# A spectral mixer with a feed-forward network: eight places for the first units' rows, the last pairs' table in six transfers, two splits moved

## The chip, the cores and the metric

The kernel runs on one core of a Trainium2 chip. The metric is the device time of one execution in microseconds. PE is the matmul engine (TensorE), DVE VectorE, ACT ScalarE, POOL GpSimd and SP SyncE, which only issues transfers. ACT and POOL issue transfers as well.

## The reference

Two parts follow each other. The first takes x (4 batches, 3008 positions, 256 channels) through a real Fourier transform over the positions, mixes the channels with a complex matrix, shrinks the result and goes back. The second is a feed-forward network with 2048 hidden units on the 12032 rows.

```python
X = np.fft.rfft(x, axis=1)
Yr = Xr @ w_r - Xi @ w_i + b_r
Yi = Xr @ w_i + Xi @ w_r + b_i
Y = sign(Y) * maximum(abs(Y) - 0.01, 0)      # real and imaginary part each
y = np.fft.irfft(Y, n=3008, axis=1)          # as 12032 rows of 256
h = y @ w_in
out = (maximum(h, 0) + alpha * minimum(h, 0)) @ w_out
```

## The kernel before

A position is 32 a + b with a below 94 and b below 32, and the transform is done in two steps. Every float32 operand of a matmul is split into two parts, a "hi" (a copy rounded to fp32r) and a "lo" (what is left), and three matmuls (hi hi, hi lo, lo hi) stand for one product. The hi is a copy on ACT or DVE, the lo a subtraction on DVE or POOL (`rest`).

The work of one batch:

- **forward1(s)**, 16 units of two values of b: the first transform step, three matmuls of 512 columns. DVE splits x (`split_x`: a cast to x_hi, then x_lo). ACT copies the result out of PSUM (`copy_fwd`, L816) and stores it to a scratch tensor in HBM (`store_fwd`, L363). The place in SBUF that it is copied to is given by `out_place` and `out_rows`; a place is written again only when the store that last read it has landed.
- **forward2(p)**, 24 pairs: the second step on 128 rows loaded back from the scratch (`load_pair`, pair_raw), which needs all of the batch's stores. ACT makes pair_hi (`split_pair`), DVE pair_lo (`rest_pair`). The stationary operand's counterpart is the table tw_parts, one for three pairs: ACT makes its hi (`split_tw`, L825), POOL its lo (`rest_tw`, L1332).
- **mixing(p)**: 12 matmuls with the channel matrix mixw, from spec_hi (ACT, `split_spec`) and spec_lo (DVE, `rest_spec`). POOL negates a part of spec_lo.
- add_bias (DVE), find_above (ACT), shrink (DVE), then shr_hi (ACT, `split_shrunk`) and shr_lo (DVE, `rest_shrunk`); **inverse2(p)** with the table itw, copied to inv_sb by ACT (`copy_inv`) and stored.
- **inverse1(u)**: the last step, which makes y_hi and y_lo in SBUF, the input of the feed-forward network.

The network runs over 24 tiles of some 502 rows, 16 steps each (hidden, then output two steps later). Batches 1 to 3 of the first part are put between its steps. Only batch 0 has a stretch of its own, before the tiles: 16 units of forward1 up to 23 us, the 24 pairs from 32 to 96 us, then some rest of inverse work, and the tiles from 109 us on.

The order of the instructions on every engine is written out by hand, engine by engine (sync from L369, tensor, scalar, vector, gpsimd), and semaphores tie them. No planner is at work. In batch 0's stretch the order on each engine is a loop over k from -1 to 22, and in iteration k:

- PE: forward2(k+1), mixing(k), inverse2(k-2);
- ACT: copy_inv(k-3), split_spec(k+1), find_above(k-1), split_pair(k+3), split_shrunk(k-1), then at k = 0, 3, ... 18 split_tw(k/3+1) and at k = 2, 5, ... 20 split_itw;
- DVE: add_bias(k-1), rest_spec(k+1), shrink(k-1), rest_pair(k+3), rest_shrunk(k-1), then at odd k from 3 to 17 a piece of a weight's split, and at k = 19 and 21 split_x of units 16 and 17, which belong to batch 1;
- POOL: negate(k+1), then rest_tw or rest_itw.

The hand-over from forward1 to the pairs: PE runs 29 filler matmuls (`stay_warm_early`, L732, 0.24 us each, whose result nobody reads) after unit 15. SP waits for the stores of all places and then loads pairs 0 to 3. Places for the rows of units 0 to 15 are taken in turn from six (OUT_FIRST): two in staging, two in g_raw, biased and shrunk.

The table of the last two pairs: pairs 22 and 23 are not taken through HBM at the end of the first part, but multiplied directly with their rows of the inverse matrix, spread over a zeroed tile (`last_raw`, in rows). POOL zeroes it when unit 7's x is split and fills it with small transfers (`load_last`, L1391): for each of two pairs e and six values b, 4 rows of 94 numbers, 12 transfers in all. DVE then makes g_hi and g_lo from it (L1242), and after that mixw_lo and the first two pair_lo, in this order.

Of the kernel before, what the change touches and what calls it, by code (L numbers as in the profile page):

```python
# [15 lines left out]
NA, NB = 94, 32  # L16
PAIRS = (NA // 2 + 1) // 2
ROWS = 4 * PAIRS
GROUPS = PAIRS // 3
# [29 lines left out]
S_HEAD = NB // 2  # L49
# [4 lines left out]

OUT_RING, OUT_HEAD = 2, 4

OUT_FIRST = 6
HEAD_V = 3

PAIRS_END = 2  # L60

HEAD_ROWS = 4 * (PAIRS - PAIRS_END)
# [67 lines left out]
def mixer_kernel(nc, x, w_r, w_i, b_r, b_i, w_in, w_out, alpha, dft, idft, twiddles, out):  # L130
    with ExitStack() as ctx:
# [35 lines left out]
        biased = sb("biased", [P, 2, DIM])  # L167
        above = sb("above", [P, 2, DIM])
        low = sb("low", [P, 1])
        shrunk = sb("shrunk", [P, 2, DIM])  # L170
        shr_hi, shr_lo = (sb(f"shr_{h}", [P, 2, DIM], F32R) for h in ("hi", "lo"))
        inv_sb = sb("inv_sb", [P, 3, DIM])


        rows = sb("rows", [P, HEAD_V, 2 * DIM])
# [26 lines left out]
        def ffw_raw(w):  # L202
            return turned[:, w % 2, :, :, :, :].rearrange("p k b h e -> p (k b h e)")[:, 0:4 * DIM]

        h_ps = ctx.enter_context(nc.psum_tensor("h_ps", [P, 2, 512], F32))
# [29 lines left out]
        last_zero, last_hi_done, last_lo_done, end_hi_done, end_lo_done, last_loaded = (  # L235
            sem(n) for n in ("last_zero", "last_hi_done", "last_lo_done", "end_hi_done", "end_lo_done", "last_loaded"))
# [87 lines left out]
        def out_rows(s):  # L324
            k = out_place(s)
            if k >= OUT_HEAD:
                return (biased, shrunk)[k - OUT_HEAD][0:ROWS, :, :].rearrange("p q d -> p (q d)")
            return staging[:, k, :] if k < OUT_RING else g_raw[0:ROWS, k - OUT_RING, :]

        def stores_before(s, k):  # L330
# [36 lines left out]
        def _(sp):  # L367
# [29 lines left out]
            def load_pair(p):  # L397
                g, j = divmod(p, PAIRS)
                if p >= 4:
                    sp.wait_ge(pair_lo_done, p - 3)  # L400
                if j < 4:
                    for k in range(OUT_FIRST):
                        sp.wait_ge(fwd_stored[k], stores_before(S_HEAD * (g + 1), k))
                sp.dma_start(pair_raw[:, p % 4, :], fwd_pairs[g, :, j, :]).then_inc(pair_loaded[p % 4], 16)
# [90 lines left out]
            for f in range(TILES):  # L495
                for m in range(STEPS):
# [21 lines left out]
                    p = p_unit(f, m, 0)  # L518
# [3 lines left out]
                    p = p_unit(f, m, 2)  # L522
                    if p is not None and p % 3 == 0:
                        load_table(p // 3 + 1)
                    p = p_couple(f, m, 6)
# [17 lines left out]
        def _(pe):  # L543
# [186 lines left out]
            def stay_warm_early(count, ps):  # L730
                for n in range(count):
                    pe.matmul(ps, dft_hi[:, :], x_hi[:, 1, :], start=True, stop=True)  # L732
# [11 lines left out]
            pe.wait_ge(hi_const, 1)  # L744
            for s in range(S_HEAD):
                forward1(s)
            stay_warm_early(29, h_ps[:, 1, :])
            for k in range(-1, PAIRS - 1):
                forward2(k + 1)
                if k == 0:  # L750
# [32 lines left out]
            for f in range(TILES):  # L783
                for m in range(STEPS):
# [8 lines left out]
                    p = p_unit(f, m, 0)  # L793
                    if p is not None:
                        forward2(p)
                    p = p_couple(f, m, 5)
# [3 lines left out]
                    p = p_couple(f, m, 2)  # L800
                    if p is not None:
                        mix_couple(p)
                    q = f * STEPS + m - LAG
# [6 lines left out]
        def _(act):  # L810
# [7 lines left out]
            def split_tw(t):  # L818
                if t < GROUPS:
                    act.wait_ge(table_loaded[t % 2], 16 * (t // 2 + 1))  # L820
                else:
                    act.wait_ge(table_loaded[0], 16 * (GROUPS // 2 + t - GROUPS + 1))
                if t >= 2:
                    act.wait_ge(spec_mm, 3 * (t - 1))
                act.activation(tw_parts[:, t % 2, :, 0, :], table_place(t)[:, 0, :].rearrange("p (k c) -> p k c", k=3),  # L825
                               ACT.Copy).then_inc(tw_hi_done, 1)
# [64 lines left out]
            def find_above(p):  # L891
                act.wait_ge(biased_done, p + 1)
                if p >= 1:
                    act.wait_ge(shrunk_done, p)
                act.activation(above[:, 0, :], biased[:, p % 2, :], ACT.Relu, bias=low[:, :]).then_inc(above_done, 1)  # L895
# [80 lines left out]
            for k in range(-1, PAIRS - 1):  # L976
                if k >= 3:
                    copy_inv(k - 3)
                split_spec(k + 1)
                if k >= 1:  # L980
                    find_above(k - 1)
                if 2 <= k + 3 < PAIRS:
                    split_pair(k + 3)
                if k >= 1:
                    split_shrunk(k - 1)
                if k >= 0 and k % 3 == 0 and k // 3 + 1 < GROUPS:
                    split_tw(k // 3 + 1)
                if k >= 0 and k % 3 == 2 and k // 3 + 1 < GROUPS:
                    split_itw(k // 3 + 1)
            for p in (PAIRS - 2, PAIRS - 1):  # L990
# [18 lines left out]
            for f in range(TILES):  # L1009
                for m in range(STEPS):  # L1010
                    q = f * STEPS + m
# [3 lines left out]
                    p = p_unit(f, m, 0)  # L1015
# [9 lines left out]
                    p = p_couple(f, m, 5)  # L1025
                    if p is not None:
                        copy_couple(p)
                    p = p_couple(f, m, 3)
# [5 lines left out]
                    p = p_unit(f, m, -3)  # L1034
                    if p is not None:
                        split_pair(p)
                    p = p_unit(f, m, 0)
# [8 lines left out]
                    p = p_unit(f, m, 0)  # L1046
# [16 lines left out]
        def _(dve):  # L1063
# [3 lines left out]
            def split_x(s, both):  # L1067
                x_arrived(dve, s)
                if s >= 2:
                    dve.wait_ge(fwd_mm, s - 1)  # L1070
                elif s == 0:
                    dve.wait_ge(x_zero, 2)
                dve.tensor_copy(x_hi[0:NA, s % 2, :], x_place(s)).then_inc(x_hi_done, 1)  # L1073
                if both:
                    dve.wait_ge(x_hi_done, s + 1)
                    rest(x_lo[0:NA, s % 2, :], x_place(s), x_hi[0:NA, s % 2, :]).then_inc(x_lo_done, 1)
# [156 lines left out]
            for s in range(S_HEAD):  # L1233
# [4 lines left out]
                if s == 6:  # L1238
                    dve.wait_ge(hi_const, 2)
                    rest(idft_parts[0:ROWS, 1, :], idft_raw[0:ROWS, 0:NA], idft_parts[0:ROWS, 0, :]).then_inc(const_split, 1)  # L1240
            dve.wait_ge(last_loaded, 16 * PAIRS_END * 2 * HEAD_V)
            dve.tensor_copy(flat(g_hi), last_raw).then_inc(last_hi_done, 1)  # L1242
            dve.wait_ge(last_hi_done, 1)
            rest(flat(g_lo), last_raw, flat(g_hi)).then_inc(last_lo_done, 1)
# [5 lines left out]
            for k in range(-1, PAIRS - 1):  # L1250
                if k == 1:
                    dve.wait_ge(bias_loaded, 32)
                if k >= 1:
                    add_bias(k - 1)
                rest_spec(k + 1)
                if k >= 1:
                    shrink(k - 1)
                if 2 <= k + 3 < PAIRS:
                    rest_pair(k + 3)
                if 1 <= k < PAIRS - 2:  # L1260
                    rest_shrunk(k - 1)
                if 3 <= k < 19 and k % 2 == 1:
                    split_ffw((k - 3) // 8, (k - 3) % 8 // 2)
                if k in (19, 21):
                    split_x(S_HEAD + (k - 19) // 2, True)
            for p in (PAIRS - 2, PAIRS - 1):
                add_bias(p)
                rest_shrunk(p - 1)
# [61 lines left out]
        def _(pool):  # L1330
# [54 lines left out]
                rest(wout_lo[:, w, :, :].rearrange("p m e -> p (m e)"), ffw_raw(w)[:, 2 * DIM:4 * DIM],  # L1385
                     wout_hi[:, w, :, :].rearrange("p m e -> p (m e)")).then_inc(wout_lo_done, 1)

            def load_last(e, b):

                row = HEAD_V * 2 * DIM  # L1390
                pool.dma_start(bass.AP(rows[:, :, :].tensor, b * row + (e * 2 * HEAD_V + b) * NA, [[32 * row, 4], [1, NA]]),  # L1391
                               idft[HEAD_ROWS + 4 * e:HEAD_ROWS + 4 * e + 4, 0:NA]).then_inc(last_loaded, 16)

            pool.memset(idft_parts[ROWS:P, 1, :].bitcast(F32), 0.0).then_inc(lo_zero, 1)
            pool.wait_ge(lo_zero, 1)
# [3 lines left out]
            pool.wait_ge(x_lo_done, 8)  # L1399
            pool.memset(last_raw, 0.0).then_inc(last_zero, 1)  # L1400
            pool.wait_ge(last_zero, 1)
            for e in range(PAIRS_END):
                for b in range(2 * HEAD_V):
                    load_last(e, b)
            rest_tw(0)
            rest_itw(0)
            for k in range(-1, PAIRS - 1):
# [102 lines left out]
```

## Time and profile before

| | us |
|---|---|
| median of 3 runs | 1375.19 |
| lowest, highest | 1373.89, 1375.62 |
| the profiled execution | 1378.68 |
| its span | 1376.9 |
| PE busy in the span | 1360.3 (99%) |
| DVE busy | 1026.8 (75%) |
| ACT busy | 763.7 (55%) |
| POOL busy | 327.9 (24%) |

The span runs from the first instruction of the profiled execution to its last; 1.8 us of its time lie around it. Busy shares are means over the whole: the first 110 us, batch 0's stretch, look different from the tiles.

### The profile page before, as it was taken

The page shows a single profiled execution, that of the slowest core. Times are in us where ns is not written, and L with a number is a line of the kernel's source. Part 1 is how long each engine was busy: PE and PEld are TensorE (multiplying, and loading weights), DVE is VectorE, ACT ScalarE, POOL GpSimd, SP SyncE. Part 2 cuts the span into 40 slices and gives each one's busy share as a digit, 9 for nine tenths or more (in the row PEclk, how much of TensorE's full clock was granted, in tenths as well). Part 3 has the DMA queues.
Part 4 walks back from the last instruction along what each step waited for, and adds up shares of the span by engine and source line. Part 5 has one row for each costly group of instructions (what it writes and reads, how often), then busy time and mean ns, then how long its engine had stood idle before and what let it go on. Part 6 is the DMA issues. An engine that isn't in the chain of part 4 may idle for free.

```text
span 1376.9 us, 21744 instructions
## 1 busy us (share of the span) xinstructions
PE 1360.3 (99%) x6933; PEld 1158.1 (84%) x6933; DVE 1026.8 (75%) x1892; ACT 763.7 (55%) x1711; POOL 327.9 (24%) x370
## 2 busy tenths in 40 slices
PE   8999999999999999999999999999999999999997
PEld 5998888888888888888888888888888888888886
DVE  7787788898866768989866668888886566566654
ACT  4776566666544555756644446666564444444443
POOL 4534542232201422323300332233220000000000
PEclk9999999999999999999999999999999999999999
DMA  8554523231211541323312333223211021102101
GB/s 264 168 173 139 173 68 92 70 92 54 52 44 46 144 117 58 86 70 83 78 30 50 87 108 84 72 74 81 85 43 44 26 50 39 25 26 50 27 15 16
DMA packets 174896, 106.82 MB, mean 78 GB/s; under 512 B 112442, under 2 KB 150586, under 8 KB 174783
## 3 DMA queue, kind: packets, MB, share of 16 engines
q1 hardware_dynamic: 170344, 101.58, 27.4%
q10 hardware_dynamic: 3959, 3.70, 0.8%
q8 instruction: 56, 0.92, 0.3%
q14 instruction: 57, 0.47, 0.1%
q0 software_dynamic: 480, 0.16, 0.1%
HBM read 67.89 MB, written 37.49 MB: 77 GB/s over the span
## 4 chain that ended last, share of the span: by engine, by line
PE 93%; DVE 2%; ACT 2%; issue 1%; POOL 1%; DMA 1%; SPq 0%; POOLq 0%; ACTq 0%; DVEq 0%
PE out_ps L546 39%; PE h_ps L546 38%; PE work_ps L546 10%; PE work_ps L657 2%; PE work_ps L589 2%; PE work_ps L659 1%; ACT above L895 1%; PE work_ps L590 1%; DVE shrunk L1135 1%; POOL rows L1391 0%; SPq L381 0%; ACT shr_hi L901 0%; DMA rows<-in_idft_dram 0%; DMA rows<-in_x_dram 0%; DVE biased L1127 0%
## 5 line engine op out<-in xcount | busy, mean ns | idle before, releaser
L934 ACT ACTIVATE rows<-h_ps 128x502 f32<-128x502 f32 (+1 forms) x384 | 225.3, 587 | 510.3 <-PE h_ps L546 510.3
L1166 DVE SCALAR_TENSOR_TENSOR g_raw<-rows,keep,h_ps 128x502 f32<-128x502 f32 (+1 forms) x384 | 280.3, 732 | 264.6 <-ACT rows L934 261.3
L546 PE MATMUL out_ps<-g_hi,wout_hi 128*128 128x502 f32 (+1 forms) x768 | 305.0, 397 | 0.2
L546 PE MATMUL h_ps<-y_hi,win_hi 128*128 128x502 f32 (+1 forms) x768 | 300.0, 391 | 1.2 <-DVE g_raw L1166 1.0
L546 PE MATMUL out_ps<-g_hi,wout_lo 128*128 128x502 f32 (+1 forms) x768 | 299.8, 390 | 0.0
L546 PE MATMUL h_ps<-y_lo,win_hi 128*128 128x502 f32 (+1 forms) x768 | 299.7, 390 | 0.0
L546 PE MATMUL out_ps<-g_lo,wout_hi 128*128 128x502 f32 (+1 forms) x768 | 299.0, 389 | 0.0
L546 PE MATMUL h_ps<-y_hi,win_lo 128*128 128x502 f32 (+1 forms) x768 | 298.9, 389 | 0.0
L1065 DVE TENSOR_TENSOR g_lo<-g_raw,g_hi 128x502 fp32r<-128x502 f32 (+1 forms) x384 | 268.4, 699 | 1.8 <-ACT g_hi L943 1.4
L943 ACT ACTIVATE g_hi<-g_raw 128x502 fp32r<-128x502 f32 (+1 forms) x384 | 237.0, 617 | 6.7 <-DVE g_raw L1166 6.2
L546 PEld LDWEIGHTS h_ps<-y_hi,win_hi 128*128 128x128 f32 x768 | 145.0, 189 | 32.1 <-issue 2.0
L546 PEld LDWEIGHTS h_ps<-y_hi,win_lo 128*128 128x128 f32 x768 | 144.4, 188 | 30.7
L546 PEld LDWEIGHTS out_ps<-g_hi,wout_lo 128*128 128x128 f32 x768 | 144.8, 189 | 29.9
L546 PEld LDWEIGHTS h_ps<-y_lo,win_hi 128*128 128x128 f32 x768 | 144.7, 188 | 29.5
L546 PEld LDWEIGHTS out_ps<-g_hi,wout_hi 128*128 128x128 f32 x768 | 145.0, 189 | 23.1 <-DVE g_lo L1065 1.0
L546 PEld LDWEIGHTS out_ps<-g_lo,wout_hi 128*128 128x128 f32 x768 | 145.5, 189 | 22.2
L1332 POOL TENSOR_TENSOR back_lo<-inv_sb,back_lo 128x256 fp32r<-128x256 f32 x61 | 54.4, 892 | 414.0 <-ACT back_lo L920 413.9
L1354 POOL TENSOR_TENSOR room<-room 128x128 f32<-128x128 f32 x72 | 60.0, 834 | 322.6 <-DVE room L1089 322.6
L1332 POOL TENSOR_TENSOR x_lo<-x_raw,x_hi 94x512 fp32r<-94x512 f32 x44 | 59.0, 1340 | 83.0 <-DVE x_hi L1073 83.0
L546 PE MATMUL work_ps<-mixw_hi,spec_hi 128*128 128x256 f32 x216 | 61.5, 285 | 0.0
L546 PE MATMUL work_ps<-mixw_lo,spec_hi 128*128 128x256 f32 x216 | 61.0, 282 | 0.0
L546 PE MATMUL work_ps<-mixw_hi,spec_lo 128*128 128x256 f32 x216 | 60.9, 282 | 0.0
(177 smaller groups left out, 2032.2 us busy)
## 6 DMA issues: line engine op xcount, KB each, us to landing
pair_raw<-fwd_scratch SPq DMA_DIRECT2D x96, 128.0 KB, 2.2
rows<-inv_scratch SPq DMA_DIRECT2D x61, 192.0 KB, 2.4
table<-in_twiddles_dram SPq DMA_DIRECT2D x28, 384.0 KB, 3.5
inv_scratch<-inv_sb SPq DMA_DIRECT2D x36, 256.0 KB, 2.2
x_raw<-in_x_dram SPq DMA_DIRECT2D x56, 160.0 KB
fwd_scratch<-staging SPq DMA_DIRECT2D x46, 192.0 KB, 2.1
inv_sb<-inv_scratch SPq DMA_DIRECT2D x122, 64.0 KB, 2.3
out_dram<-turned SPq DMA_DIRECT2D x124, 40.0 KB, 1.8
```

What stands on the lines that cost most here:

```text
L546: mm = pe.matmul(ps, lhs, rhs, start=(first and n == 0), stop=(last and n == len(terms) - 1), **kw)
L589: pe.matmul(both, hi, tw.rearrange("p w c -> p (w c)"), start=True, stop=False, skip_group_check=True)
L590: mm = pe.matmul(both[:, 0:P], lo, tw[:, 0, :], start=False, stop=True, skip_group_check=True)
L657: pe.matmul(i_bank(u)[:, b * 2 * NA:(b + 1) * 2 * NA], back_hi[:, v % 2, d], parts, start=b == 0, stop=False, skip_group_check=True)
L659: pe.matmul(i_views(u)[0], back_lo[:, v % 2, h * P:(h + 1) * P], idft_rest[:, :, :], start=False, stop=True, skip_group_check=True).then_i ...
L895: act.activation(above[:, 0, :], biased[:, p % 2, :], ACT.Relu, bias=low[:, :]).then_inc(above_done, 1)
L934: act.activation(negpart[:, q % 2, 0:size], h_ps[:, q % 2, 0:size], ACT.Relu, scale=-1.0).then_inc(negpart_done, 1)
L943: act.activation(g_hi[:, q % 3, 0:size], g_raw[:, q % 2, 0:size], ACT.Copy).then_inc(g_hi_done, 1)
L1065: return dve.tensor_tensor(dst, whole, hi.bitcast(F32), ALU.subtract)
L1166: dve.scalar_tensor_tensor(g_raw[:, q % 2, 0:size], negpart[:, q % 2, 0:size], keep[:, m:m + 1], h_ps[:, q % 2, 0:size], ALU.mult, ALU.add ...
L1332: return pool.tensor_tensor(dst, whole, hi.bitcast(F32), ALU.subtract)
L1354: pool.tensor_tensor(spec_sum, spec[:, :, 0, :], spec[:, :, 1, :], ALU.add).then_inc(sum_done, 1)
```

## The change

Five edits, all in batch 0's stretch.

```diff
-OUT_FIRST = 6
+OUT_FIRST = 8
@@ out_rows
-                return (biased, shrunk)[k - OUT_HEAD][0:ROWS, :, :]...
+                return (biased, shrunk, above, inv_sb)[k - OUT_HEAD][0:ROWS, 0:2, :]...
@@ load_pair
-                if j < 4:
+                if j == 0:
                     for k in range(OUT_FIRST):
                         sp.wait_ge(fwd_stored[k], stores_before(S_HEAD * (g + 1), k))
@@ tensor
-            stay_warm_early(29, h_ps[:, 1, :])
+            stay_warm_early(27, h_ps[:, 1, :])
@@ scalar, the loop over k
+                if k >= 0 and k % 3 == 0 and k // 3 + 1 < GROUPS:
+                    split_tw(k // 3 + 1)
                 if 2 <= k + 3 < PAIRS:
                     split_pair(k + 3)
                 if k >= 1:
                     split_shrunk(k - 1)
-                if k >= 0 and k % 3 == 0 and k // 3 + 1 < GROUPS:
-                    split_tw(k // 3 + 1)
@@ vector
-            dve.wait_ge(last_loaded, 16 * PAIRS_END * 2 * HEAD_V)
+            dve.wait_ge(last_loaded, 16 * 2 * HEAD_V)
...
-                if k in (19, 21):
-                    split_x(S_HEAD + (k - 19) // 2, True)
+                if k in (18, 20):
+                    split_x(S_HEAD + (k - 18) // 2, True)
@@ gpsimd
-            def load_last(e, b):
+            def load_last(b):
                 row = HEAD_V * 2 * DIM
-                pool.dma_start(bass.AP(rows[:, :, :].tensor, b * row + (e * 2 * HEAD_V + b) * NA, [[32 * row, 4], [1, NA]]),
-                               idft[HEAD_ROWS + 4 * e:HEAD_ROWS + 4 * e + 4, 0:NA]).then_inc(last_loaded, 16)
+                pool.dma_start(bass.AP(rows[:, :, :].tensor, b * row + b * NA, [[32 * row, 4], [2 * HEAD_V * NA, PAIRS_END], [1, NA]]),
+                               idft[HEAD_ROWS:HEAD_ROWS + 4 * PAIRS_END, 0:NA].rearrange("(e r) a -> r e a", e=PAIRS_END)
+                               ).then_inc(last_loaded, 16)
@@
-            for e in range(PAIRS_END):
-                for b in range(2 * HEAD_V):
-                    load_last(e, b)
+            for b in range(2 * HEAD_V):
+                load_last(b)
```

Units 0 to 15 take their places in turn from eight; the two new ones lie in above and in the first two thirds of inv_sb. SP checks the places' stores once per batch, ahead of pair 0, as it issues in order. Units 16 and up keep the four and two places that they had. The last pairs' table moves the same 48 rows in six transfers of eight rows. PE has two fillers fewer. On ACT the table's split of an iteration stands ahead of the pair's and of shr_hi. The x splits of units 16 and 17 are done one iteration earlier.

## Rows read from the trace of the kernel before

**Rows 1.** Busy time by windows: length, engines' busy time (instructions), granted clock, DMA share, GB/s.

```profile
29.90:31.90 2.00, 0.00 (x0) 0.03 (x1) 2.00 (x3) 0.76 (x2) 0.44 (x1) 1.00 0.91 219
31.90:36.00 4.10, 4.10 (x17) 3.81 (x18) 1.70 (x5) 2.12 (x7) 0.93 (x2) 0.52 0.90 308
...
90.00:96.00 6.00, 5.09 (x41) 4.78 (x40) 4.72 (x13) 3.69 (x12) 2.30 (x4) 1.00 0.40 128
...
150.00:700.00 550.00, 550.00 (x2854) 472.87 (x2853) 447.42 (x818) 324.58 (x737) 158.32 (x179) 1.00 0.30 79
```

**Rows 2.** PE's waits over the whole run: total us, times, longest.

```profile
PE h_ps L546 <- DVE pair_lo L1065: 2.1, 1, 2.1
...
PE h_ps L546 <- POOL tw_parts L1332: 0.8, 2, 0.5
```

**Rows 3.** The chain that ended last, 0 to 70 us: start, us, what.

```profile
15.14 6.59 POOL rows L1391 x11
21.73 4.91 DMA rows<-in_idft_dram
...
27.44 2.04 DVE g_lo L1065
...
66.10 0.62 PE h_ps L546 x6
66.72 1.47 PE out_ps L546 x12
```

**Rows 4.** Timeline, 22 to 40 us: start, us, engine, line, what [idle before].

```profile
22.69 0.39 PE L546 MATMUL work_ps<-x_hi,dft_lo 128*128 128x512 f32 x1
...
22.93 6.90 PE L732 MATMUL h_ps<-x_hi,dft_hi 128*128 128x512 f32 x29
24.29 0.59 ACT L816 ACTIVATE g_raw<-work_ps 96x512 f32<-96x512 f32 x1 [1.63 <-DMA fwd_scratch<-g_raw]
24.92 0.31 ACTq L363 DMA_DIRECT2D fwd_scratch<-g_raw  x1
...
27.78 1.99 SPq L404 DMA_DIRECT2D pair_raw<-fwd_scratch  x4
28.25 2.09 POOL L1332 TENSOR_TENSOR itw_lo<-table,itw_hi 128x384 fp32r<-128x384 f32 x1
29.82 0.42 ACT L838 ACTIVATE pair_hi<-pair_raw 128x256 fp32r<-128x256 f32 x1 [2.66 <-DMA pair_raw<-fwd_scratch]
...
31.90 0.54 PE L546 MATMUL h_ps<-tw_parts,pair_hi 128*128 128x128 f32 x2 [2.07 <-DVE pair_lo L1065]
...
39.20 0.33 PE L546 MATMUL out_ps<-mixw_hi,spec_hi 128*128 128x256 f32 x1
```

**Rows 5.** Timeline, POOL's three output stores at the end.

```profile
1370.56 2.09 POOL L356 DMA_DIRECT2D out_dram<-turned  x3 [74.59 <-DVE turned L1226]
```

**Rows 6.** Transfers issued at 22.69, then at 24.92: KB, us from issue to landing.

```profile
fwd_scratch<-g_raw ACTq DMA_DIRECT2D x1, 192.0 KB, 4.4
...
fwd_scratch<-g_raw ACTq DMA_DIRECT2D x1, 192.0 KB, 2.6
```

**Rows 7.** Timeline around 62 us: POOL's table subtraction and PE behind it.

```profile
61.90 1.43 POOL L1332 TENSOR_TENSOR tw_parts<-table,tw_parts 128x384 fp32r<-128x384 f32 x1 [0.56 <-ACT tw_parts L825]
...
63.38 0.44 PE L546 MATMUL h_ps<-tw_parts,pair_hi 128*128 128x128 f32 x2 [0.49 <-POOL tw_parts L1332]
```

**Rows 8.** Timeline, 86 to 96 us: spec_lo(20) and mixing(20), the x splits, PE's wait.

```profile
86.00 0.42 DVE L1065 TENSOR_TENSOR spec_lo<-h_ps,spec_hi 128x256 fp32r<-128x256 f32 x1 [0.36 <-ACT spec_hi L846]
...
87.13 0.34 PE L546 MATMUL out_ps<-mixw_hi,spec_hi 128*128 128x256 f32 x1
...
87.65 0.42 DVE L1073 CAST x_hi<-x_raw 94x512 fp32r<-94x512 f32 x1
...
93.84 0.69 DVE L1065 TENSOR_TENSOR x_lo<-x_raw,x_hi 94x512 fp32r<-94x512 f32 x1
...
95.25 0.39 PE L546 MATMUL out_ps<-mixw_hi,spec_hi 128*128 128x256 f32 x1 [0.91 <-DVE spec_lo L1065]
```

More of the change, by code:

```diff
@@ L326, in out_rows @@
             if k >= OUT_HEAD:
-                return (biased, shrunk)[k - OUT_HEAD][0:ROWS, :, :].rearrange("p q d -> p (q d)")
+                return (biased, shrunk, above, inv_sb)[k - OUT_HEAD][0:ROWS, 0:2, :].rearrange("p q d -> p (q d)")
             return staging[:, k, :] if k < OUT_RING else g_raw[0:ROWS, k - OUT_RING, :]
```

## The prediction

> **What bounds the kernel now.** I first read the busy time by stretches. From 150 to 700 us PE is busy for all 550 us [rows 1], so a microsecond gained or lost ahead of that is worth a microsecond at the end, and no edit can gain anything inside. The edits lie before 100 us. There the waits of PE name two things: one wait of 2.1 us on DVE's pair_lo, and two waits, 0.8 us together, on POOL's tw_parts [rows 2]. The reader should see a third in the windows: after the 2.1 us of idle PE the granted clock is 0.52, the lower level (1.2 GHz), until some time before 39 us, while in 90 to 96 us PE idles 0.91 us and the clock stays at 1.00, 2.4 GHz [rows 1].
>
> The chain of waits says what ends the 2.1 us: POOL issues transfers of the last pairs' table, 11 of them in 6.59 us; the last lands 4.91 us after its issue; then DVE makes g_hi, g_lo (2.04) and mixw_lo and only then pair_lo [rows 3]. But a second chain ends little earlier, and the timeline shows it: unit 15's copy on ACT waits 1.63 us for an older store (unit 9's, its place being the same), its own store is issued at 24.92, SP can load pair 0 at 27.78, ACT splits it from 29.82 to 30.24 [rows 4]. Had DVE been free, PE would have started near 30.24 + 0.35 (pair_lo) + 0.15 = 30.75 instead of 31.90. Both must be shortened to gain more than 1.15.
>
> **Part 1: six transfers for twelve.** POOL's issue costs 6.59 / 11 = 0.60 each [rows 3]. A transfer now has twice the rows. The trace shows no such form; the nearest is POOL's three output stores, 2.09 / 3 = 0.70 each for 40 KB pieces in far more runs [rows 5]. I take 0.6 (bounds 0.56 and 1.2, twice the price for twice the rows). The sixth is issued at 15.14 + 5 x 0.60 = 18.1 and lands at 18.1 + 4.9 = 23.0. From landing to PE the chain took 31.90 - 26.64 = 5.26, so DVE allows PE to start at 28.3; with 1.2 each it is 15.14 + 6.0 + 4.9 + 5.3 = 31.3. At 0.6 DVE drops out and the stores' chain is last.
>
> **Part 2: eight places.** PE ends unit 15 at 22.69 + 0.39 = 23.08. Unit 15 now reuses no place younger than unit 7's, so ACT copies it at 23.15 instead of 24.29 and issues the store at 23.8 instead of 24.92. The tempting sum is 1.15 us earlier for everything behind. Against it stand the landings: unit 14's store is issued at 22.69 and lands 4.4 us later, at 27.1; unit 15's is issued at 24.92 and lands after 2.6, at 27.5 [rows 4, 6]. They land in order, 0.4 apart, so unit 15's already stood behind unit 14's work on the last of the DMA engines. Unit 14's issue is not moved. So the last landing is between 27.1 and 27.5 (outer bound 26.4, if 2.6 us held from 23.8); I take 27.3. SP, which waited 0.26 from landing to issue and checked six semaphores ahead of each of four loads, now checks eight once: pair 0 issued at about 27.45, the next three closer together. The known rest is the same, 31.90 being replaced by 30.75 for a free DVE: PE starts at 30.75 - 0.33 = 30.4, say 30.5. That is 1.4 us earlier than 31.90.
>
> The ACT work behind the copy (mixw_hi, the tables) comes 1.1 us earlier too and DVE's mixw_lo with it: no new wait. That above and inv_sb serve as places costs nothing, since ACT writes them next only for pairs that are loaded after all stores.
>
> **Part 3: 27 fillers for 29.** 29 took 6.90 us [rows 4], so 27 end at 22.93 + 6.42 = 29.35. They were never on the path. PE is then idle from 29.35 to 30.5, 1.15 us, instead of 2.07. Which clock does it meet? The rows show 1.00 kept over 0.91 idle and lost over 2.07 [rows 1]. 1.15 is much nearer the first: I take the full clock. What it gives: from PE's start to the first matmul of mixing(1) it took 39.20 - 31.90 = 7.30 at mostly the lower clock [rows 4]. At full clock the same work is three forward2 at 0.62, one mixing at 1.47 [rows 3] and three fillers at 6.90 / 29 = 0.24: 4.1, with the first-matmul gaps 4.2. The feeding engines keep up: of 4.10 us in that stretch ACT was busy for 2.12, DVE for 1.70 and POOL for 0.93 [rows 1]. Gain 7.3 - 4.2 = 3.1. Bounds: 0 (clock lost all the same) and 3.1.
>
> **Part 4: tw_parts split ahead of the pair's.** It happens for seven tables, at pairs k = 0, 3, ... 18. At k = 9 POOL subtracts from 61.90 for 1.43 us and PE starts 0.49 late at 63.38 [rows 7]; the other of the two waits is the rest of the 0.8, 0.27 us. Two ACT instructions now come behind the table's instead of ahead of it, so POOL can use the 0.56 us that it idled there [rows 7]: it starts at 61.34 and ends by 62.8, and PE wants it at 63.38 - 0.49 = 62.9. Both waits go: 0.76 us. In exchange pair_hi and shr_hi come up to 0.4 later. pair_hi is used two pairs on. shr_hi delays DVE's last subtraction of the pair and with it add_bias and rest_spec of the next; rest_spec has 0.7 us in hand there in a pair without other DVE work: spec_lo(20) was made from 86.00 to 86.42, and PE came to it at 87.13 [rows 8]. Cost 0; bounds 0 and 0.3 for each of the three pairs with a weight split too, so the term is between 0 and 0.76.
>
> **Part 5: x splits at k = 18 and 20 instead of 19 and 21.** One is a cast of 0.42 and a subtraction of 0.69 [rows 8], at the end of DVE's work for a pair. At 21 it stood straight ahead of spec_lo(23), and PE idled 0.91 for it at 95.25 [rows 8]. At 19 (87.65) no idle. At 18 it meets the late shr_hi. Put in behind rest_shrunk with 0.42 + 0.69, it ends at about 86.5 by my following of DVE's order, and add_bias and spec_lo(20) behind it end at 87.15 where PE wants it at 87.13 [rows 8]: +0.1 of idle. At 20, ACT also has the inverse table, and find_above(20) stands behind DVE's late add_bias in ACT's order, ahead of spec_hi(23). Followed in the same way (an estimate from DVE's 0.42 an instruction and ACT's order): spec_lo(22) some 0.5 us after PE wants it, and spec_lo(23) at 95.1. So most of the 0.91 comes back as two new stalls; I take +0.2 gained, bounds -0.5 and +0.9.
>
> A DVE subtraction of 1128 elements took 2.04 us beside POOL's itw_lo, itself 2.09 [rows 3, 4], where 0.69 for 512 [rows 8] would make 1.5. The Trainium skill says why (SBUF — State Buffer, section "SBUF: two separate sides"): VectorE and GpSimd hold one port pair exclusively, and the loser blocks for the whole instruction. Parts 4 and 5 put POOL's subtraction beside more DVE subtractions; by the rule in full, rest_pair at k = 18 would wait out POOL's 1.0 us, and part 5 would come out at -0.1 instead of +0.2. It isn't put into the sum.
>
> **Sum.** 1.4 + 3.1 + 0.76 + 0.2 = 5.5 us. The profiled execution took 1378.68 (span 1376.9 and 1.8 around it, untouched): 1373.2. The three runs' median, 1375.19, is 3.5 below the profiled time; the same 5.5 off it gives 1369.7, my forecast.
>
> **Rivals.**
> *The last stores do land 1.1 us earlier.* For it: the last store alone needed 2.6 us; against it the landings 27.1 and 27.5 in order [rows 4, 6]. PE starts at 29.6 and all else holds: 6.4 gained, 1368.8.
> *The clock is lost in spite of the shorter gap.* For it: 1.15 is longer than any gap that kept it in these rows. Then only 1.4 + 0.76 + 0.2 = 2.4: 1372.8.
> *The table's six transfers cost 1.0 to 1.3 each.* DVE's chain ends last again, PE starts near 31.3, after 1.95 us of idle, at the lower clock: 0.6 + 1.0 gained, 1373.6.
> *Slower: they cost more still.* Twice the rows written by POOL at four times the price, 2.2 us each, while DVE's x splits run beside. The sixth lands at 15.14 + 11 + 4.9 = 31.0, PE starts at 36.3, 4.4 late, less 1.0: 3.4 slower, 1378.6. PE's start is later than now from 1.32 us for a transfer on, and the whole slower from about 1.5. Against it: 0.60 and 0.70 are all that POOL shows.
>
> **Chances.** Forecast 0.57 (its own range 1368.9 to 1371), early stores 0.12, clock lost 0.18, dear transfers 0.09, slower 0.04. A change under 0.2% (2.75 us) can't be told from none by a measurement of this kernel: the second and third rival fall there, and a part of the first case if part 5 turns out at -0.5 and the clock returns late. Faster 0.70, same 0.26, slower 0.04. Range 1368.2 to 1373.4, which leaves out the dearest transfers and double luck.
>
> **What would show it.** In the profile after: POOL's six issues done by 19 and g_hi started near 23; unit 15's copy at 23.15 without a wait; the last store landing at 27.1 to 27.5 although issued at 23.8; PE starting at 30.5 with a clock of 1.0; no wait on tw_parts; new waits of some tenths on spec_lo near the end of the pairs in place of the one of 0.91. A PE start before 30, or a clock under 1.0 in the 5 us after it, would prove the sum wrong by those terms.

## The result and the profile after

| us | before | after |
|---|---|---|
| median of 13 runs each, same chip | 1375.62 | 1378.85 |
| lowest, highest | 1373.89, 1379.53 | 1378.10, 1381.46 |
| profiled execution | 1378.68 | 1378.49 |
| its span | 1376.9 | 1376.3 |

The ratio after to before is 1.0023, 95% interval 1.0015 to 1.003: the changed kernel is slower by 3.2 us, at 1378.85 where 1369.7 was forecast, and outside the stated range of 1368.2 to 1373.4. The two profiled executions don't show this loss (1378.68 and 1378.49), because the one of before lies 3.1 us above its kernel's median; the section on the clock comes back to that.

The first view is again the busy time by windows, now of the changed kernel (columns as in [rows 1]).

```profile
29.90:31.90 2.00, 2.00 (x15) 1.84 (x16) 0.74 (x3) 1.17 (x5) 0.07 (x1) 1.00 0.91 317
31.90:36.00 4.10, 4.10 (x37) 4.10 (x36) 2.66 (x7) 2.56 (x8) 2.86 (x4) 1.00 1.00 314
...
90.00:96.00 6.00, 4.93 (x39) 4.50 (x38) 4.89 (x11) 3.42 (x11) 2.18 (x3) 1.00 0.44 121
...
150.00:700.00 550.00, 550.00 (x2854) 472.85 (x2853) 448.13 (x820) 324.48 (x736) 157.09 (x178) 1.00 0.30 79
```

The start is what was forecast: from 29.90 on PE is busy, at the full clock, with 37 matmuls in the 4.10 us that held 17 before. From 150 us nothing differs. The loss must lie between. PE's waits over the whole run of the changed kernel name it:

```profile
PE work_ps L546 <- DVE shr_lo L1065: 2.5, 5, 0.7
...
PE out_ps L546 <- DVE spec_lo L1065: 1.5, 2, 1.0
...
PE h_ps L546 <- DVE pair_lo L1065: 0.8, 1, 0.8
```

The wait on pair_lo is down from 2.1 to 0.8 and that on tw_parts is gone [rows 2], but five waits on shr_lo are new, and spec_lo has two where it had one of 0.9. The timeline of the changed kernel's start:

```profile
14.93 3.87 POOL L1391 DMA_DIRECT2D rows<-in_idft_dram  x6 [0.31 <-POOL rows L1401]
...
22.84 0.59 ACT L816 ACTIVATE inv_sb<-work_ps 96x512 f32<-96x512 f32 x1 [0.46 <-PE work_ps L546]
23.46 0.31 ACTq L363 DMA_DIRECT2D fwd_scratch<-inv_sb  x1
24.46 0.75 DVE L1242 CAST g_hi<-rows 128x1128 fp32r<-128x1128 f32 x1 [2.44 <-DMA rows<-in_idft_dram]
...
26.50 2.04 DVE L1065 TENSOR_TENSOR mixw_lo<-turned,mixw_hi 128x1024 fp32r<-128x1024 f32 x1
26.57 1.77 SPq L404 DMA_DIRECT2D pair_raw<-fwd_scratch  x4
...
29.14 0.91 DVE L1065 TENSOR_TENSOR pair_lo<-pair_raw,pair_hi 128x256 fp32r<-128x256 f32 x2 [0.60 <-ACT pair_hi L838]
...
29.84 0.41 PE L546 MATMUL h_ps<-tw_parts,pair_hi 128*128 128x128 f32 x2 [0.76 <-DVE pair_lo L1065]
...
33.99 0.34 PE L546 MATMUL out_ps<-mixw_hi,spec_hi 128*128 128x256 f32 x1
```

Against [rows 4]: six issues take 3.87 us (0.65 each), unit 15's copy has no wait on a store, SP loads at 26.57 and not 27.78, PE starts at 29.84 and not 31.90, and mixing(1) at 33.99 and not 39.20. DVE is through with mixw_lo at 28.54 and then waits 0.60 us for pair_hi, so the chain that ends last is now the loaded pair's and not DVE's. 5.2 us are won by mixing(1).

One table carries the rest: the start of the first matmul of mixing(k), read from PE's timeline in each trace. The kernel e1_head_only (below) has the new start and both splits at their old places.

| start of mixing(k), us | before | after | e1_head_only |
|---|---|---|---|
| 1 | 39.20 | 33.99 | 34.05 |
| 7 | 53.53 | 48.43 | 48.38 |
| 14 | 71.57 | 68.53 | 66.41 |
| 19 | 84.33 | 82.06 | 79.17 |
| 23 | 95.25 | 94.68 | 90.06 |
| 1 to 23 | 56.05 | 60.69 | 56.01 |

Of 5.21 us won at mixing(1), 0.57 is left at mixing(23), and the spans differ by 0.6. The other 4.64 are lost inside the loop. Up to mixing(7) hardly anything goes (14.44 us from mixing(1), 14.33 in e1_head_only), although two tables are split by then. After that the loss comes in steps of 0.2 to 1.3 us, in the pairs just behind an iteration that splits a table or x, and the last pair gives 0.7 back.

What happens in such an iteration, from the changed kernel's timeline at k = 6, k = 9, and at the x split of k = 20 (L1065 is the line of every `rest`, whose two operands are named behind the arrow; PSUM is the memory that the matmuls write, and h_ps, out_ps and work_ps lie in it):

```profile
48.81 1.02 POOL L1332 TENSOR_TENSOR tw_parts<-room,tw_parts 128x384 fp32r<-128x384 f32 x1
49.07 1.04 DVE L1065 TENSOR_TENSOR pair_lo<-pair_raw,pair_hi 128x256 fp32r<-128x256 f32 x1 [0.19 <-ACT pair_hi L838]
50.04 0.41 DVE L1065 TENSOR_TENSOR shr_lo<-shrunk,shr_hi 128x256 fp32r<-128x256 f32 x1
50.51 0.39 PE L546 MATMUL work_ps<-shr_hi,itw_hi 128*128 128x256 f32 x1 [0.45 <-DVE shr_lo L1065]
...
57.42 1.23 POOL L1332 TENSOR_TENSOR tw_parts<-table,tw_parts 128x384 fp32r<-128x384 f32 x1
57.70 1.23 DVE L1065 TENSOR_TENSOR shr_lo<-shrunk,shr_hi 128x256 fp32r<-128x256 f32 x1
...
89.95 1.17 POOL L1332 TENSOR_TENSOR itw_lo<-room,itw_hi 128x384 fp32r<-128x384 f32 x1 [0.99 <-ACT itw_hi L831]
90.28 1.39 DVE L1065 TENSOR_TENSOR x_lo<-x_raw,x_hi 94x512 fp32r<-94x512 f32 x1
91.93 0.40 DVE L1065 TENSOR_TENSOR spec_lo<-h_ps,spec_hi 128x256 fp32r<-128x256 f32 x1
92.39 0.39 PE L546 MATMUL out_ps<-mixw_hi,spec_hi 128*128 128x256 f32 x1 [0.99 <-DVE spec_lo L1065]
```

POOL starts its subtraction first; the next DVE subtraction with two operands in SBUF takes 1.04 or 1.23 us in place of 0.41, and ends 0.28 us after POOL's. PE's matmul behind it is late. x_lo takes 1.39 in place of 0.69, in the same way. In all three cases the end is POOL's end plus the subtraction's usual time, less 0.13 or 0.14 us: these times say that DVE stood still until POOL was done, and did not merely run slower.

### The profile page after: what moved, and what is told of

Read it like the earlier page. It is cut to its first block, busy times and chain, and to the rows that moved or that the text cites. A ratio compares the mean times of both kernels' runs of the same rounds, so it can differ in the third digit from the quotient of the medians.

```text
span 1376.3 us, 21701 instructions
## 1 busy us (share of the span) xinstructions
PE 1359.1 (99%) x6931; PEld 1155.6 (84%) x6931; DVE 1028.6 (75%) x1892; ACT 763.7 (55%) x1711; POOL 322.5 (23%) x364
## 4 chain that ended last, share of the span: by engine, by line
PE 94%; DVE 2%; ACT 1%; issue 1%; DMA 1%; POOL 0%; SPq 0%; POOLq 0%; DVEq 0%; ACTq 0%
PE out_ps L546 39%; PE h_ps L546 38%; PE work_ps L546 11%; PE work_ps L657 2%; PE work_ps L589 2%; PE work_ps L659 1%; PE work_ps L590 1%; DVE x_hi L1073 0%; DVE x_lo L1065 0%; DMA pair_raw<-in_x_dram 0%; SPq L381 0%; ACT above L895 0%; DVE biased L1127 0%; DVE shrunk L1135 0%; DVE shr_lo L1065 0%
## 5 line engine op out<-in xcount | busy, mean ns | idle before, releaser
L1065 DVE TENSOR_TENSOR g_lo<-g_raw,g_hi 128x502 fp32r<-128x502 f32 (+1 forms) x384 | 267.4, 696 | 1.8 <-ACT g_hi L943 1.4
```

What stands on the lines that cost most here:

```text
L1065: return dve.tensor_tensor(dst, whole, hi.bitcast(F32), ALU.subtract)
```

## The experiments

Medians are compared with runs of the kernel before on the same chip (e1 to e4 on one chip, e5 to e11 on another). "1 to 23" is the time from mixing(1) to mixing(23), as in the table.

### Which part loses it

**e1_head_only**: the changed kernel with both splits back.

```diff
@@ scalar: split_tw(k // 3 + 1) again behind split_pair and split_shrunk
-                if k in (18, 20):
-                    split_x(S_HEAD + (k - 18) // 2, True)
+                if k in (19, 21):
+                    split_x(S_HEAD + (k - 19) // 2, True)
```

> The changed kernel with both moved splits put back (the table's behind shr_hi, the x splits at k = 19 and 21); eight places, six transfers and 27 fillers stay. Theory A (the head gains, the moved splits lose all of it, and the before kernel loses its clock in some executions only): the timed runs are 1.5 to 3 us faster than before (the 5.2 us by which PE reaches mixing(1) earlier, less the 3.1 us of clock that most executions of before do not lose), PE idles 0.9 us at the last spec_lo as before. Theory B (the profiled execution of before is a typical one, and it is timing without the profiler that differs): 4.5 to 5.5 us faster than before. Rival C (the head's gain is itself given back later in the tiles): within 1 us of before.

Measured 1374.42 (11 runs) against 1375.97, ratio 0.9989 (0.998 to 0.9998); 1 to 23 is 56.01, that of before. The median is 1.55 us below before's, the lower end of what theory A expected. The profiled execution took 1373.84 (span 1371.7). The moved splits cost the 4.6 us between the spans. At k = 6 this kernel shows

```profile
48.57 0.42 DVE L1065 TENSOR_TENSOR shr_lo<-shrunk,shr_hi 128x256 fp32r<-128x256 f32 x1 [0.15 <-ACT shr_hi L901]
48.91 0.42 DVE L1127 TENSOR_TENSOR biased<-out_ps,bias 128x256 f32<-128x256 f32 x1
49.04 1.02 POOL L1332 TENSOR_TENSOR tw_parts<-room,tw_parts 128x384 fp32r<-128x384 f32 x1 [0.99 <-ACT tw_parts L825]
49.69 0.42 DVE L1065 TENSOR_TENSOR spec_lo<-h_ps,spec_hi 128x256 fp32r<-128x256 f32 x1 [0.36 <-ACT spec_hi L846]
```

At the old place POOL's subtraction stands beside biased and spec_lo, which have an operand in PSUM, and both take 0.42 us, their usual time. The old order was hiding it.

**e2_tw_back**: only the table's split back, x left at 18 and 20. **e3_x_back**: only the x splits back, the table's left early.

```diff
e2  @@ scalar: split_tw(k // 3 + 1) again behind split_shrunk(k - 1)
e3  @@ vector
-                if k in (18, 20):
-                    split_x(S_HEAD + (k - 18) // 2, True)
+                if k in (19, 21):
+                    split_x(S_HEAD + (k - 19) // 2, True)
```

> The changed kernel with only the table's split put back behind shr_hi. Theory A (POOL's table subtraction now runs beside DVE's shr_lo and holds it up once per three pairs): no shr_lo longer than 0.6 us among the pairs, the two PE waits on tw_parts (0.8 us) return, and the kernel is 2 to 3 us faster than the changed one. If the x splits at 18 and 20 alone were the loss: no faster than the changed one by more than 0.5 us.

> The changed kernel with only the x splits put back at k = 19 and 21. Theory A: the stalls of PE on shr_lo once per three pairs stay (0.4 to 0.7 us each), the two on spec_lo at 86 and 92 us (0.48 and 0.99) become smaller and one of some 0.9 at the last pair returns: 0.5 to 1.7 us faster than the changed kernel. If the order of the x splits makes no difference: within 0.4 us of the changed kernel.

e2: 1375.35, ratio 0.9995 (0.9987 to 1.0004), 1 to 23 is 57.12: the moved x splits cost 1.1. No shr_lo of e2 in the loop takes more than 0.43, the waits on the table are back (1.0 us in PE's waits), and the kernel is 3.5 us below the changed one where 2 to 3 were expected. e3: 1378.13, ratio 1.0017 (1.0008 to 1.0025), 1 to 23 is 60.47: the moved table splits cost 4.5. Together they cost 4.7 and not 5.6: where the table's split is early too, x_lo at k = 18 runs behind POOL's subtraction and takes 0.69. By the medians e3 gains 0.7 us over the changed kernel, as expected (0.5 to 1.7); by 1 to 23 it is only 0.2. In e3 PE's waits hold the five of the changed kernel:

```profile
PE work_ps L546 <- DVE shr_lo L1065: 2.5, 5, 0.7
```

and in e2 both x splits stand beside a POOL subtraction:

```profile
80.98 1.17 POOL L1332 TENSOR_TENSOR tw_parts<-room,tw_parts 128x384 fp32r<-128x384 f32 x1 [0.99 <-ACT tw_parts L825]
81.31 1.38 DVE L1065 TENSOR_TENSOR x_lo<-x_raw,x_hi 94x512 fp32r<-94x512 f32 x1
...
83.41 0.39 PE L546 MATMUL out_ps<-mixw_hi,spec_hi 128*128 128x256 f32 x1 [0.33 <-DVE spec_lo L1065]
...
87.57 1.38 DVE L1065 TENSOR_TENSOR x_lo<-x_raw,x_hi 94x512 fp32r<-94x512 f32 x1
...
89.68 0.39 PE L546 MATMUL out_ps<-mixw_hi,spec_hi 128*128 128x256 f32 x1 [0.99 <-DVE spec_lo L1065]
```

At k = 18 POOL splits a twiddle table, at k = 20 an inverse one; at 19 and 21, where x was, it splits none.

### Is it the blocking, or ACT's order

A rival for the five waits: shr_hi is later on ACT, and shr_lo with it, whatever POOL does. **e5_after_tw3** is the changed kernel with POOL's table subtraction in three instructions; if a whole instruction blocks DVE, a shorter one blocks it for less.

```diff
-                rest(tw_parts[:, t % 2, :, 1, :], table_place(t)[:, 0, :]..., ...).then_inc(tw_lo_done, 1)
+                for j in range(3):
+                    op = rest(tw_parts[:, t % 2, j, 1, :], table_place(t)[:, 0, j * P:(j + 1) * P], tw_parts[:, t % 2, j, 0, :])
+                op.then_inc(tw_lo_done, 1)
```

> The changed kernel with POOL's table subtraction cut into three instructions of 128 columns; order and waits as they are. If POOL's instruction holds a port that DVE's shr_lo needs, as a whole (the block theory): DVE can slip in after a third, the longest shr_lo falls from 1.24 us to 0.8 or less, PE's five waits on shr_lo (2.5 us) fall under 1 us, and the kernel is 1 to 2.5 us faster than the changed one. If it is a later shr_hi on ACT that delays shr_lo (the price that the prediction gave): shr_lo as long as before and no gain.

Measured 1378.02, ratio 1.0017 (1.0008 to 1.0027): 2.1 us above before, where the changed kernel was 3.2 above. The longest shr_lo falls from 1.23 to 0.68, and the five waits on it (2.5 us) to one of 0.3, though ACT's order is that of the changed kernel. Timeline at k = 6 and PE's waits of this kernel:

```profile
48.92 1.66 POOL L1332 TENSOR_TENSOR tw_parts<-room,tw_parts 128x128 fp32r<-128x128 f32 x3
49.59 0.68 DVE L1065 TENSOR_TENSOR shr_lo<-shrunk,shr_hi 128x256 fp32r<-128x256 f32 x1
```

```profile
PE out_ps L546 <- DVE spec_lo L1065: 1.7, 2, 1.0
...
PE h_ps L546 <- POOL tw_parts L1332: 1.1, 2, 0.6
```

The block decides the waits on shr_lo. But 1 to 23 falls only from 60.69 to 59.24: three instructions take POOL 1.66 us between DVE's, so PE now waits 1.1 for the table. The time fell by 0.8 to 1.1 us (the median alone, or against before on its chip), at the lower edge of the 1 to 2.5 expected, and in 1 to 23 a loss of 3.2 us against e1 stays, 1.1 of it the x splits'; how the rest divides between the later shr_hi, the shortened blocks and the table's waits was not tried.

### Which part wins at the start

**e6_six_transfers** and **e7_eight_places** have one part of the new start each, splits back, 27 fillers.

```diff
e6  -OUT_FIRST = 8
    +OUT_FIRST = 6
e7  @@ gpsimd: load_last(e, b) for 2 x 6 transfers of 4 rows again
```

> Six places, six transfers, 27 fillers, moved splits put back: of the head's edits only the table's transfers. Unit 15's copy waits for unit 9's store and its store is issued near 24.9 and lands near 27.5, pair 0 is loaded near 27.6 and PE starts near 30.7 (before: 31.90). Mixing(1) near 35 if the clock is kept, near 38 if it is lost in this execution. Rival (the transfers alone give all): PE starts at 29.8 as in the changed kernel.

> Eight places, twelve transfers, 27 fillers, moved splits put back: of the head's edits only the places. The stores land near 26.5 as in the changed kernel, but DVE gets g_hi only when the twelfth transfer lands near 26.6, and PE starts at 31.5 to 32, after more than 2 us of idle. Rival (the DVE chain has slack): PE starts at 29.8 to 30.5.

e6, one execution: 1373.77 (span 1371.8). Its start:

```profile
23.70 0.60 ACT L816 ACTIVATE g_raw<-work_ps 96x512 f32<-96x512 f32 x1 [1.41 <-DMA fwd_scratch<-g_raw]
24.33 0.31 ACTq L363 DMA_DIRECT2D fwd_scratch<-g_raw  x1
...
26.63 1.77 SPq L404 DMA_DIRECT2D pair_raw<-fwd_scratch  x4
...
29.82 0.41 PE L546 MATMUL h_ps<-tw_parts,pair_hi 128*128 128x128 f32 x2 [0.83 <-DVE pair_lo L1065]
```

Unit 15's store is issued 0.87 later than in the changed kernel, and SP's load stands 0.06 later, PE's start 0.02 earlier. My expectation for this kernel was wrong and its rival right: in this execution the two further places won nothing. e7, one execution: 1378.23 (span 1376.4), and the old start:

```profile
26.45 1.08 DVE L1242 CAST g_hi<-rows 128x1128 fp32r<-128x1128 f32 x1 [4.46 <-DMA rows<-in_idft_dram]
...
31.23 0.66 PE L546 MATMUL h_ps<-tw_parts,pair_hi 128*128 128x128 f32 x2 [2.17 <-DVE pair_lo L1065]
```

With twelve transfers DVE's chain is last again, PE stands idle for 2.17 us and the granted clock in 31.90 to 36.00 is 0.50. PE's start is 0.3 us earlier than the 31.5 to 32 that I expected. So in these two executions the start is won by the six transfers. There is one execution of each, and landings vary by as much as 2 us (last section), so a gain of some tenths by the places, in other executions, is not excluded.

### Is the clock in the time of a usual run

**e4_before_fill37** is the kernel before with more fillers, which leave PE 0.5 us idle and start pair 0 no earlier; **e8_head_fill29** is e1 with two fillers more.

```diff
e4  -            stay_warm_early(29, h_ps[:, 1, :])
    +            stay_warm_early(37, h_ps[:, 1, :])
e8  -            stay_warm_early(27, h_ps[:, 1, :])
    +            stay_warm_early(29, h_ps[:, 1, :])
```

> The kernel before with 37 fillers for 29, so that PE idles some 0.2 us instead of 2.07 ahead of pair 0 and nothing else is changed. Theory A (the lower clock after the gap costs 3.1 us, but only in some executions): the profile shows a clock of 1.0 from 32 to 39 us and mixing(1) 3 us after where it would be, at 36.2 instead of 39.2; every timed run has a mean clock of 0.999 or so; the median is 0 to 1.5 us under before's and the spread is narrower at the top (none above 1377). Theory B (all executions of before lose it): 3 us faster than before. Rival (the gap is not what lowers the clock): clock again near 0.5 after 32 us, same time as before.

> Eight places, six transfers and 29 fillers, moved splits put back (the first experiment with two fillers more). PE ends its fillers at 29.85, about when pair 0 is ready, so PE starts at 29.85 to 29.95 as with 27. If the idle of 0.6 us there still cost the clock in some executions: the slow tail (1376.1 to 1379.2 in 3 of 11 runs) goes and the median falls by 0 to 0.5 us, to 1373.9 to 1374.4. If those runs lose the clock elsewhere: the same tail again.

e4: 1375.21 (1374.39 to 1375.84), ratio 0.9993 (0.9984 to 1.0001). Its windows and PE's start:

```profile
31.90:36.00 4.10, 4.10 (x34) 3.94 (x35) 2.14 (x6) 2.13 (x7) 1.48 (x3) 1.00 0.91 270
```

```profile
31.78 0.41 PE L546 MATMUL h_ps<-tw_parts,pair_hi 128*128 128x128 f32 x2 [0.46 <-DVE pair_lo L1065]
```

PE starts at the same time as before, but mixing(1) follows 4.15 us behind that start and not 7.30: in the profile the clock alone is worth 3.1 us (span 1376.9 to 1373.8). Yet the median moves by 0.8, which the interval doesn't tell from nothing. The executions of before fall in two groups by the mean granted clock over the span. In the runs beside e1 to e4, 19 of 35 stand at .998 or more with 1374.0 to 1376.8 us, and 16 at .997 or less with 1376.0 to 1379.1. In the other two sets of runs of before 8 of 19 and 18 of 27 are at .997 or less. All eleven of e4 are of the first kind and at its level. So it appears that about half of the executions of before have the stretch at the lower clock, and the profiled one, at .996, was among the dearest. The new start isn't free of it: 3 of 13 executions of the changed kernel (1380.6 to 1381.5) and 3 of 11 of e1 (1376.1 to 1379.2) are at .997 or less. Among the executions at .998 or more the medians are 1375.2 for before and for e4, 1378.7 for the changed kernel and 1373.9 for e1. There the new start is worth 1.3 us.

e8: 1374.78, ratio 0.9998 (0.9989 to 1.0008), and 4 of 10 executions at .997 or less, up to 1378.73, the profiled one among them. The slow executions that I expected to go did not. The profiled one shows how the new start, too, can lose the clock:

```profile
28.05 1.06 ACT L970 ACTIVATE mixw_hi<-turned 128x1024 fp32r<-128x1024 f32 x1 [4.76 <-DMA turned<-in_w_i_dram]
28.44 1.77 SPq L404 DMA_DIRECT2D pair_raw<-fwd_scratch  x4
...
31.66 0.66 PE L546 MATMUL h_ps<-tw_parts,pair_hi 128*128 128x128 f32 x2 [2.25 <-DVE pair_lo L1065]
```

Up to here the program is that of the changed kernel, but mixw's rows land 4 us later and the stores 1.9. The landings vary from one execution to the next, and two fillers more don't cover 2.25 us.

### A version that beats both

**e9_head_thirds** is e8 with POOL's table subtraction in thirds at the old place and PE waiting for its own third; **e10_head_thirds_x** adds one move of a cast; **e11_head_thirds33** is e9 with 33 fillers.

```diff
e9  @@ forward2(p)
-                if k == 0:
-                    pe.wait_ge(tw_lo_done, p // 3 + 1)
+                pe.wait_ge(tw_lo_done, p + 1)
    @@ rest_tw
+                for j in range(3):
+                    rest(tw_parts[:, t % 2, j, 1, :], ...).then_inc(tw_lo_done, 1)
e10 @@ vector: unit 17's x_hi cast at k = 20, its x_lo at k = 21 as before
e11 @@ tensor: stay_warm_early(33, ...)
```

> The new start (eight places, six transfers, 29 fillers), both splits at their late pairs, but POOL's subtraction for a table in three instructions of 128 columns, and TensorE waits for its pair's own third. If the last waits of the loop on the table (0.7 us in two pairs in e1_head_only) come from the length of POOL's subtraction, they go and no new wait on VectorE comes, since the instructions still run at the old place: mixing(1) to mixing(23) falls from 56.01 to about 55.3, and the median lies 0.5 to 0.8 us below e1_head_only's 1374.42 in executions that keep the clock, near 1373.8. Rival: three instructions take POOL's port longer in sum (about 0.68 x 3 against 1.22) and block as much VectorE work elsewhere: no gain, 1374.4 or more.

> The same, and of unit 17's x split the cast one pair earlier (pair 20), with the subtraction left at pair 21. In before's trace the wait ahead of the last pair's first matmul (0.9 us) hung on spec_lo, which ran behind x_lo. If the cast was a part of what is late, mixing(22) to mixing(23) (3.03 in e1_head_only) falls by up to 0.4 and the time with it, to about 1373.4. Rival: the cast on the crowded earlier pair delays shr_hi there as the whole split did (1.1 us in e2_tw_back): the time is that of e9_head_thirds or up to 0.5 above it.

> e9_head_thirds with 33 fillers instead of 29, which end about 0.9 us later, near 30.5. In executions whose table rows land early this costs 0.3 to 0.9 us; in those in which they land late (the start of pair 0 at 31.66 in e8_head_fill29) TensorE stands idle for 1.2 us and not 2.25 and keeps the full clock, which takes the upper tail away: all executions within 1.5 us, median 0.3 to 0.9 above e9_head_thirds, mean the same or lower. Rival: the tail has another cause than the idle time ahead of pair 0, and 3 or 4 of the executions still show a mean clock of .997 or less.

| 11 runs each; before 1376.69 | median | lowest, highest | ratio (interval) | 1 to 23 | at clock .997 or less |
|---|---|---|---|---|---|
| e9 | 1374.67 | 1373.78, 1376.86 | 0.9984 (0.9976 to 0.9993) | 56.40 | 1 |
| e10 | 1374.42 | 1373.26, 1374.82 | 0.9982 (0.9973 to 0.9991) | 56.18 | 0 |
| e11 | 1374.44 | 1373.99, 1376.32 | 0.9985 (0.9976 to 0.9994) | 56.39 | 0 |

All three beat both kernels, by 2.0 to 2.3 us against before, whose median is 0.7 to 0.8 higher in this set than in the others (18 of its 27 executions are at .997 or less); part of the margin is that they keep the clock. The thirds did not help: e9's 56.40 is above e1's 56.01. The table's waits go (mixing(10) to (11) is 2.80 for 3.22), but pair 21, 2.45 in e1, takes 3.04:

```profile
81.12 1.30 POOL L1331 TENSOR_TENSOR tw_parts<-room,tw_parts 128x128 fp32r<-128x128 f32 x3 [0.99 <-ACT tw_parts L824]
...
85.39 0.39 PE L546 MATMUL out_ps<-mixw_hi,spec_hi 128*128 128x256 f32 x1 [0.29 <-DVE spec_lo L1064]
```

so the rival's result, no gain, came. Counted from mixing(1), DVE's shr_lo ahead of this stands 0.3 later than in e1 and PE's mixing(19) 0.2 earlier, so PE came early to a DVE that was late; what made DVE late was not settled. e10's cast brings 0.2 of the hoped 0.4 and its median, 1374.42 where 1373.4 was hoped for, is not told apart from e9's. e11's fillers are not told apart from e9's by the median, which was expected 0.3 to 0.9 above it; its spread is 2.3 us and not 1.5. None of its executions lost the clock, but with 29 fillers only 1 of 22 of e9 and e10 did, so the four fillers more aren't shown to have done it. e9's own profile shows PE idle for 1.15 us ahead of pair 0 and the clock at 1.00 behind it. None of the three is told apart from e1 by these runs, which were made on another chip.

## Why the prediction was wrong

- **Part 1, six transfers**: right. 0.65 an issue for the 0.6 taken; the table lands later than forecast (g_hi at 24.46, forecast near 23), and DVE's chain, with g_lo at 1.33 and not 2.04, still left 0.60 us to spare.
- **Part 2, eight places**: the landing was mis-sized. The last store landed 3.0 us after its issue, at 26.5, and not at 27.3; the outer bound was 26.4. PE started at 29.84 for 30.5. That is the rival of the early stores in time, not in cause: e6 has the old places and the same start. The argument that the issue doesn't set the landing held; that the landing would stay at 27.3 did not, since landings move by one or two microseconds between executions (SP's load at 26.57 to 28.60 in these traces).
- **Part 3, the clock**: right in the trace. Kept over 0.76 us of idle (and 1.15 in e9), pair 0 to mixing(1) took 4.15 us, forecast 4.2. With parts 1 and 2 the start brought 5.2 us in the profile (before to e1: span 1376.9 to 1371.7), for 4.5 forecast.
- **The sum**: the first step that failed is "the same 5.5 off it gives 1369.7". It took a term of one execution off a median of executions of which about half seem to lack it: the profiled one was 3.5 above the median shown, about what the clock stretch costs (3.1 in e4). Parts 1 to 3 give e1 1.55 us in the median, not 4.5. Taken off the profiled time they make 1374.2, and e1's profiled execution took 1373.84.
- **Part 4**: the step that failed by most is "Cost 0; bounds 0 and 0.3 for each of the three pairs with a weight split too". Both waits on tw_parts went, 0.76 as worked out. But shr_hi's delay was all that was looked for, and POOL's earlier start ahead of DVE's two subtractions of that iteration was not. It cost 4.5 us net over seven tables (e3), a mean of 0.64 but unevenly: 0.1 for the first two together in the changed kernel (0.5 in e3), 0.6 to 0.7 for those of k = 6 and 12. Five waits on shr_lo of 0.4 to 0.7 are 2.5 us of it; the one between mixing(10) and (11) takes the place of the table's own wait there (3.54 for 3.21). The rest is in shorter stalls of the pairs around them, as mixing(11) to (12), 2.68 for 2.46.
- **Part 5**: "+0.2" was -1.1 (e2), past its lower bound of -0.5. The 0.99 at mixing(22) and the 0.33 to 0.48 at mixing(20) were seen as stalls of 0.5 and 0.1; x_lo was priced at 0.69, its time with no POOL subtraction beside it, and took 1.38 in both places in e2.

Of the miss of 9.15 us these account for 9.0: 5.7 for parts 4 and 5 together (4.7 lost in place of 0.96 gained), 2.9 for the start (1.55 us in the median for 4.5), and 0.4 because before's median of 13 runs is above that of the first three.

In parts 4 and 5 the missing cost stood in the rows, as g_lo at 2.04 [rows 3]. The prediction put it beside POOL's itw_lo, which is misread: itw_lo starts 0.8 us after g_lo. From the timeline of before:

```profile
26.83 1.45 POOL L1332 TENSOR_TENSOR tw_parts<-table,tw_parts 128x384 fp32r<-128x384 f32 x1 [4.54 <-ACT tw_parts L825]
...
29.40 2.02 DVE L1065 TENSOR_TENSOR mixw_lo<-turned,mixw_hi 128x1024 fp32r<-128x1024 f32 x1
```

What held g_lo (27.44) was POOL's tw_parts, which runs to 28.28; 1.33 behind that, g_lo's time in the changed kernel, gives 29.6, and it ended at 29.48. Then itw_lo, which started at 28.25 behind g_lo's start, was held in its turn: it took 2.09 us where it takes 1.01 beside nothing (e6). And mixw_lo, which takes 1.22 in e6, waited for itw_lo and took 2.02. So some 1.5 us of DVE's chain ahead of pair 0 in the kernel before were the same effect. In e6, where neither was held up, PE started at 29.82 all the same, since it waited for the loaded pair. What a start with twelve transfers would gain by moving POOL's two subtractions was not tried.

The Trainium skill (SBUF — State Buffer, section "SBUF: two separate sides") says that the shared port pair is an exclusive lock between a GpSimd operation that reads SBUF and a VectorE one with two SBUF inputs, and that whichever starts first holds it for its whole instruction. The traces agree, in both directions: 1.23 for shr_lo beside POOL's 1.23, 1.39 for x_lo beside 1.17, 2.09 for POOL's itw_lo behind g_lo, and 0.42 for biased and spec_lo, one operand in PSUM, beside 1.02. The prediction quoted the rule, applied it once, to one rest_pair, and left it out of the sum. Applied to each of the moved instructions it would have said: DVE later by 0.6 to 0.8 for each of seven tables and by 0.7 for each x split. How much of that reaches PE depends on how far DVE is ahead: at k = 3 shr_lo takes 1.23 too, and PE loses 0.1.

The one rival that ended slower (transfers at four times the price) had the wrong mechanism. No rival had the moved splits lose.

## What to carry to other kernels

When a GpSimd operation on SBUF is moved, list the VectorE operations that it will stand beside, and price each with two SBUF operands at the whole GpSimd instruction; beside DVE's operations with one operand in PSUM it cost nothing here. Look which of the two starts first: that one runs at its usual time and the other waits. An order that looks merely late may be there for that. Before a stall or a clock stretch of a profile is taken off a median, see whether the profiled execution stands at the median: if it is above, the stretch may be what makes it so. When landings ahead of a start vary, cover PE with fillers up to the late ones: in the kernel before, none of 11 executions lost the clock with 37 fillers, and about half seem to with its own 29.

## What the runs showed that was not expected

The last landings ahead of pair 0 differ by 2 us between executions of nearly the same program (SP's load at 26.57 in the changed kernel, 28.44 in e8, 28.60 in e4), and idle times of 2.07, 2.17 and 2.25 us went with a clock of 0.52, 0.50 and 0.50 behind them, those of 0.46, 0.76 and 1.15 with 1.00 (nothing between 1.15 and 2.07 was measured). This fits the two groups of the kernel before: its 29 fillers end at a fixed time, and how long PE is idle behind them is left to the landings. It was not shown execution by execution, since only one of each kernel is profiled. Three subtractions of 128 columns on POOL took 1.66 us beside DVE's subtractions, 1.30 at another pair, where one of 384 took 1.02.
